# Gathering and scaling the next job's token rows at another place of a mixture-of-experts job loop

## What is computed

```python
x = attention(q, k, v, g_q, g_k)              # 4 batches, 12 heads, 448 tokens, 64 wide
x = x.transpose(0, 2, 1, 3).reshape(1792, 768)
# top-1 mixture of experts, 8 experts
expert = argmax(normalised(x) @ normalised(emb).T / tau); gate = softmax(...)[expert]
y = gate * (relu(x @ w1[expert]) @ w2[expert])   # w1: 768 x 1024, w2: 1024 x 768
# gated layer
out = (sigmoid(y @ w_gate) * (y @ w_val)) @ w_out
```

## Time and profile before

| | |
|---|---|
| median of 3 runs | 1223.03 us (1221.73 to 1224.38) |
| the profiled execution | 1228.75 us, its span 1227.2 us |
| TensorE (PE) busy | 1149.4 us, 94% of the span |
| VectorE (DVE), ScalarE (ACT), GpSimd (POOL) | 54%, 47%, 28% |
| attention to about 331 us, experts to about 669 us, layer 2 to the end | |

### The profile page before, as it was taken

One profiled execution on the slowest core, in us unless ns is written; L12 is line 12 of the kernel. 1 busy time (PEld: TensorE's weight loads), 2 busy tenths in 40 slices (PEclk: granted clock), 3 DMA queues, 4 the chain that ended last, 5 costly groups with the idle time before them and its releaser, 6 DMA issues. The chain is left out here.

```text
span 1227.2 us, 22232 instructions
## 1 busy us (share of the span) xinstructions
PE 1149.4 (94%) x7464; PEld 1005.1 (82%) x7465; DVE 658.5 (54%) x1136; ACT 576.8 (47%) x1282; POOL 347.9 (28%) x305
## 2 busy tenths in 40 slices
PE   4899999999669998999998999999999999999996
PEld 3566666666359998999998999999999999999995
DVE  4777777777755655565666343333333343333332
ACT  3777777777235544454555333233323333233321
POOL 7586767672362234323440000010001000010001
PEclk9999999999869999999999999999999999999998
DMA  3133432321157666766766434344333433343431
GB/s 80 36 103 99 123 95 72 89 62 46 23 134 198 185 175 164 193 186 179 205 181 161 132 103 111 105 140 117 112 103 111 139 103 103 103 147 105 117 105 51
DMA packets 255845, 147.12 MB, mean 120 GB/s; under 512 B 11128, under 2 KB 253048, under 8 KB 255808
## 3 DMA queue, kind: packets, MB, share of 16 engines
q1 hardware_dynamic: 251008, 132.25, 38.9%
q0 software_dynamic: 3872, 14.38, 4.1%
q10 hardware_dynamic: 928, 0.00, 0.0%
HBM read 135.52 MB, written 11.09 MB: 119 GB/s over the span
## 5 line engine op out<-in xcount | busy, mean ns | idle before, releaser
L1561 POOL DMA_INDIRECT out_dram<-rows,idp x16 | 18.0, 1125 | 561.6 <-DVE rows L1525 557.9
L1516 DVE TENSOR_TENSOR gv<-vb,sg 128x448 f32<-128x448 f32 x48 | 30.0, 625 | 219.8 <-PE vb L1579 203.8
L1349 PE MATMUL hb<-XH,W1H 128*128 128x256 f32 (+1 forms) x384 | 112.6, 293 | 16.4 <-issue 9.3
L727 ACT ACTIVATE PR<-sc,negmax 112x448 f32<-112x448 f32 x192 | 122.1, 660 | 0.0
L476 DVE TENSOR_REDUCE negmax<-sc 112x2 f32<-112x896 f32 x96 | 100.8, 1086 | 27.2 <-PE sc L836 26.9
L1349 PE MATMUL yb<-HH,W2H 128*128 128x256 f32 (+1 forms) x384 | 112.9, 294 | 0.0
L1472 ACT ACTIVATE l_WH<-stream 128x768 fp32r<-128x768 f32 x100 | 82.1, 839 | 62.3 <-PE vb L1579 60.9
L1577 PE MATMUL gb<-YH,l_WH 128*128 x288 | 107.1, 372 | 3.8 <-DVE l_WL L1509 3.6
L1351 PE MATMUL hb<-XH,W1L 128*128 128x256 f32 (+1 forms) x384 | 110.5, 288 | 0.0
L1350 PE MATMUL hb<-XL,W1H 128*128 128x256 f32 (+1 forms) x384 | 110.4, 288 | 0.0
L1350 PE MATMUL yb<-HL,W2H 128*128 128x256 f32 (+1 forms) x384 | 109.6, 285 | 0.0
(11 more groups left out here) (228 smaller groups left out, 2809.1 us busy)
## 6 DMA issues: line engine op xcount, KB each, us to landing
raw<-in_moe_w_dram SPq DMA_DIRECT2D x68, 384.0 KB, 4.8
stream<-in_moe_w_dram SPq DMA_DIRECT2D x48, 512.0 KB, 4.3
stream<-in_moe_w_gate_dram SPq DMA_DIRECT2D x34, 384.0 KB, 3.5
stream<-in_moe_w_val_dram SPq DMA_DIRECT2D x34, 384.0 KB, 4.1
stream<-in_moe_w_out_dram SPq DMA_DIRECT2D x32, 384.0 KB, 3.9
l_raw<-in_moe_w_gate_dram SPq DMA_DIRECT2D x16, 384.0 KB, 3.6
l_raw<-in_moe_w_val_dram SPq DMA_DIRECT2D x16, 384.0 KB, 4.2
l_raw<-in_moe_w_out_dram SPq DMA_DIRECT2D x16, 384.0 KB, 3.8
```

Source lines behind the costliest of these rows:

```text
L727: nc.scalar.activation(PR[:, h, j, :], sc[j % 2][0:P, h, 0:S], ACT.Exp, bias=negmax[:, s, j, h:h + 1], accum_out=den[:, s, h, j:j + 1]).th ...
L1349: nc.tensor.matmul(out[:, 0:n], WH[:, slot, k, :], mh, start=(k == 0), stop=False)
L1516: nc.vector.tensor_tensor(gv[:, f % 2, :], vb[f % 2][:, 0:S], sg[:, f % 2, :], ALU.mult).then_inc(prod, 1)
```

## The change

1. End of attention: VectorE builds the two matrices of the first of the four last tiles, then makes the gates, then builds the matrices of the other three.
2. SyncE waits, ahead of its first weight loads of job 0, until the rows of job 0 are turned.
3. The scaling of later jobs' rows goes from GpSimd to ScalarE (parts 0, 2) and VectorE (parts 1, 3), as a step `scale(j + 1)` between the last `h_out` and y 0. GpSimd keeps the index copy, the gathers and `store_ids`.
4. GpSimd waits, ahead of the index copy, until h 2 of job j is done too.
5. TensorE turns blocks 0 and 1 after y 0, block 2 after y 1, to block 5 after y 4; `x_out` moves likewise.

```diff
 finish():
-                for i in range(EARLY, TILES):
-                    chunk_of(i).then_inc(r.hi_l, 1)
-                    line_of(i).then_inc(r.lo_l, 1)
+                chunk_of(EARLY).then_inc(r.hi_l, 1)
+                line_of(EARLY).then_inc(r.lo_l, 1)
                 dve.wait_ge(r.exp_out, 1)
                 chain(nc.vector.tensor_reduce(r.gsum[:, :], r.EX[:, :, :], AX.X, ALU.add))
                 chain(nc.vector.tensor_scalar(r.gsum[:, :], r.gsum[:, :], 1e-9, None, ALU.add))
                 nc.vector.reciprocal(r.gate[:, :], r.gsum[:, :]).then_inc(r.gated, 1)
+                for i in range(EARLY + 1, TILES):
+                    chunk_of(i).then_inc(r.hi_l, 1)
+                    line_of(i).then_inc(r.lo_l, 1)
 SyncE:
-            rest_of(0, expert_of(sp, 1), 0)
+            following = expert_of(sp, 1)
+            sp.wait_ge(x_turned, KD)
+            rest_of(0, following, 0)
 job_order (ScalarE, VectorE):
-            x_out(j + 1, 0)
-            x_out(j + 1, 1)
+            scale(j + 1)
             for d in range(F2):
                 if d + 2 < F2:
                     w2_split(j, d + 2, 0)
                     w2_split(j, d + 2, 1)
                 y_out(j, d)
-                if d + 2 < F2:
-                    x_out(j + 1, d + 2)
+                if d == 0:
+                    x_out(j + 1, 0)
+                if d + 1 < F2:
+                    x_out(j + 1, d + 1)
                 if d in (3, 4):
                     w1_split(j + 1, d - 3)
 GpSimd:
                 pool.wait_ge(x_turned, KD * (j + 1))
                 pool.wait_ge(ids_out, 16 * (j + 1))
+                pool.wait_ge(h_done, SPLIT + F1 * j + 3)
...
                 fetch_rows(nc, c, x_rows)
                 store_ids(j + 1)
-                for a in range(4):
-                    pool.wait_ge(c.x_got[a], 16 * (j + 2))
-                    pool.sem_inc(x_arrived, 1)
-                    scale_rows(nc.gpsimd, a).then_inc(x_in, 1)
 ScalarE (VectorE alike, with a in (1, 3) and tensor_scalar):
+            def scale(j):
+                for a in (0, 2):
+                    act.wait_ge(c.x_got[a], 16 * (j + 1))
+                    nc.scalar.activation(xr[0:R, a, 0:DM], xr[0:R, a, 0:DM], ACT.Copy,
+                                         scale=xr[0:R, a, DM:ROW]).then_inc(gated_act, 1)
 TensorE:
                 if kd == 0:
-                    pe.wait_ge(x_in, 4 * j)
+                    pe.wait_ge(gated_act, 2 * (j + 1))
+                    pe.wait_ge(gated_dve, 2 * (j + 1))
...
-                turn(j + 1, 0)
-                turn(j + 1, 1)
                 for d in range(F2):
                     y(j, d, n)
-                    if d + 2 < KD:
-                        turn(j + 1, d + 2)
+                    if d == 0:
+                        turn(j + 1, 0)
+                    if d + 1 < KD:
+                        turn(j + 1, d + 1)
```

More of the change, by code:

```diff
@@ L1039, in experts @@
         yb = [ps(f"yb{i}", [128, 512]) for i in range(3)]
-        x_in = sem("x_in")
         raw1_in, raw2_in, w1_hi, w1_lo = c.raw1_in, c.raw2_in, c.w1_hi, c.w1_lo
@@ L1054, in experts @@
         x_asked = sem("x_asked")
-        x_arrived = sem("x_arrived")
         ids_out = sem("ids_out")
@@ L1132, in splits, with job_order @@
             return (count // ring) * j + (f // ring + 1)
-        def job_order(w1_split, w2_split, h_out, x_out, y_out, j):
+        def job_order(w1_split, w2_split, h_out, scale, x_out, y_out, j):
             for f in range(F1):
@@ L1155, in experts @@
         first_banks = tx + yb + hb[1:2]
-        def scale_rows(eng, a):
-            return eng.tensor_scalar(xr[0:R, a, 0:DM], xr[0:R, a, 0:DM], xr[0:R, a, DM:ROW], None, ALU.mult)
         @block.gpsimd
@@ L1218, in _ @@
             n_jobs = jobs(act, act.wait_ge)
-            for a in (0, 2):
-                act.wait_ge(c.x_got[a], 16)
-                nc.scalar.activation(xr[0:R, a, 0:DM], xr[0:R, a, 0:DM], ACT.Copy, scale=xr[0:R, a, DM:ROW]).then_inc(gated_act, 1)
+            def scale(j):
[3 more added lines that the diff above has]
+                                         scale=xr[0:R, a, DM:ROW]).then_inc(gated_act, 1)
+            scale(0)
             for kd in range(KD):
@@ L1229, in y_out @@
                     nc.scalar.activation(c.YH[:, d, bass.ds(s, T)], yb[d % YB][:, 0:T], ACT.Copy).then_inc(y_hi, 1)
-                job_order(w1_split, w2_split, h_out, x_out, y_out, j)
+                job_order(w1_split, w2_split, h_out, scale, x_out, y_out, j)
         @block.vector
@@ L1313, in _, with scale @@
             n_jobs = jobs(dve, dve.wait_ge)
-            for a in (1, 3):
-                dve.wait_ge(c.x_got[a], 16)
-                scale_rows(nc.vector, a).then_inc(gated_dve, 1)
+            def scale(j):
+                for a in (1, 3):
+                    dve.wait_ge(c.x_got[a], 16 * (j + 1))
+                    nc.vector.tensor_scalar(xr[0:R, a, 0:DM], xr[0:R, a, 0:DM], xr[0:R, a, DM:ROW], None,
+                                            ALU.mult).then_inc(gated_dve, 1)
+            scale(0)
             for kd in range(KD):
```

## The result

The change makes the kernel slower: 1237.49 us (median, 1236.73 to 1238.15) against 1222.38 beside it, ratio 1.0124, 95% interval 1.0104 to 1.0144. Forecast were 1213.7 and a range from 1208 to 1223.5.

What follows compares the result with a forecast made beforehand. TensorE was taken as the bound, so gains had to be its gaps. Terms -4.1 + 0.8 - 0.8 - 9.4 + 4.2 = -9.3 us took the median from 1223.03 to 1213.7, range 1208 to 1223.5.

Steps and rivals of the forecast that it cites:

- the rows in time: Ahead of turn 0 in six short jobs: rows arrive 0.7 us late each, +4.2 us, bounds 0 and 9.6.
- W1L waits: TensorE's waits for W1L at job ends and within jobs go: -9.4 us, other bound 0.
- Rival B: Job ends: YH is late for a reason that stays (loop, branch); -0.9 us, 1222.1, no change; chance 0.14.
- Rival A: Within jobs: late signal catches h 5, W1L waits ahead of h 7, 1.3 us per short job; 1217.3, faster; chance 0.22.
- C: Within jobs: hold catches h 4, waits ahead of h 6, 3.4 us per short job; 1234.9, slower; chance 0.13.
- D: Start of the experts: it doesn't move, block entry or VectorE's job table being next; 1216.7; chance 0.06.
- Start: Start of job 0: earlier gates and held weight loads bring TensorE's last turns forward, -4.1 us, bounds -3.3 and -4.8.
- Branches: First branch, beside released weight loads: +0.8 us (0 to +1.6); job 2's end, without the burst: -0.8 (0 to -1.6).
- The scaling moved off GpSimd: Between the last h_out and y 0: ScalarE's and VectorE's scaling fits under y 0's 2.83 us and costs nothing.

Runs made afterwards that it cites:

- The start alone: Kernel before with only the gates earlier and the weight loads of job 0 held until its rows are turned: 1217.72 us, ratio 0.9971; again 0.9966.
- before_d: Kernel before, unchanged, profiled once more on a third chip, one with prompt signals: 1221.49 us in that execution, 1221.0 in the median.

## Why the prediction was wrong

The failed step is **the rows in time**, +4.2 with an upper bound of 9.6; it measured +17.5 of waiting, and the clock, which was in no term, another 5 to 6. The demand was nearly right (turn 0 wanted 13.1 us after the split's start at 358.74, forecast 13.4). The supply was not: forecast were 13.5 us to the landing and 14.1 with the scaling, measured 15.7 to the turn. Three things add up. From release to the fourth issue it took 6.4 instead of 6.1; the issues of the four gathers take 1.38, 0.90, 1.15 and 1.15 us, where 0.91 was usual. The landing took 8.5 instead of 7.4, and 8.4 in the median of all. The rest, 0.2, is from the end of the scaling to the turn. I took the median of the earlier trace rows because both places have weight loads beside them; but those rows come from the job's end. With the same gathers one block earlier (the wait for h 1) the median landing is 6.7 us; why it is 8.4 behind h 2 is not shown. The shortfall was 0.7 us a job by the forecast, and every further us counts six times.

The Trainium skill, SBUF — State Buffer, section Who interferes with whom, holds that a VectorE instruction with both inputs in SBUF stands in the way of a GpSimd instruction that reads SBUF. The index copy agrees: 0.44 us at 359.45, inside a W1L split of VectorE that starts at 359.29 and takes 1.03, where the variant without the wait has 0.18. For descriptor writing beside such an instruction the page infers no conflict. The gathers beside VectorE's splits of W1 and W2, which both have two inputs in SBUF:

```profile
360.61 0.68 DVE L1299 TENSOR_TENSOR W2L<-stream,W2H 128x512 fp32r<-128x512 f32 x1
361.34 1.03 DVE L1239 TENSOR_TENSOR W1L<-raw,W1H 128x384 fp32r<-128x384 f32 x2
...
362.66 0.68 DVE L1299 TENSOR_TENSOR W2L<-stream,W2H 128x512 fp32r<-128x512 f32 x1
363.47 1.03 DVE L1239 TENSOR_TENSOR W1L<-raw,W1H 128x384 fp32r<-128x384 f32 x2
...
364.78 0.68 DVE L1299 TENSOR_TENSOR W2L<-stream,W2H 128x512 fp32r<-128x512 f32 x1
```

A split beside a gather does not lengthen it by itself: the fast one, 362.44 to 363.34, has the W2L split of 362.66 beside it. What the three slow ones share is a split that is already under way when they start (at 360.76, 363.64 and 365.10). All the traces here together bear that out: of 254 later-job gathers with a split under way 0.15 us after their start 230 took over 1.0 us, of 385 others 42. A gather also takes its index from SBUF (`xr<-x_rows,index`), so this does not contradict the page. And it is a coincidence in time only: no run here takes the splits away.

**The clock** was not in the sum at all. In the profile of before the only half-clock stretch behind the start of the experts lay at the branch of job 2's end, so I had no row for one behind a short wait.

**W1L waits, -9.4**: right as a reading of the trace and wrong for the measurement. The term is 9.4 on late chips, 1.0 on prompt ones. The sign was there: the profiled execution stood 5.7 above the median, and I carried that over as a constant offset, where it was mostly the very term that I meant to win. Rival B, late YH as a matter of the job's end, falls: moved with the burst, the hold left y 5 and met h 0. Rival A has its mechanism on late chips, and not its time: new waits for W1L lie ahead of h 7, 0.75 to 0.8 us in five of the six short jobs and 1.45 in the sixth (forecast 1.3), but the waits for rows shrink to 12.3 us and not to nothing, and the kernel is slower, not faster. C's waits ahead of h 6 came in no trace of the changed kernel. D falls with the start.

**Start, -4.1**: right. The start alone gives 3.5 and 4.1 us by its ratios (0.9971, 0.9966). In the changed kernel's trace:

```profile
344.83 0.62 DVE L1317 TENSOR_SCALAR xr<-xr 73x768 f32<-73x768 f32 x1 [1.03 <-DMA xr<-x_rows,index]
344.90 0.29 PEld L1393 LDWEIGHTS tx<-ident,xr 73*128 73x128 f32 x2 [0.27 <-ACT xr L1218]
...
346.66 0.99 SPq L1095 DMA_DIRECT2D raw<-in_moe_w_dram  x2
```

The last turns start at 344.90, forecast 344.1; attention's last step ahead of the gates (L686) lies at 329.30 here and at 327.96 in before's trace, so this execution was 1.3 us late already.

**Branches, +0.8 and -0.8**: they measured

```profile
L1399 PEldq COMPARE_BRANCH  x8: 87/218/3763, 346.4 to 636.3; - x8
```

```profile
L1401 PEldq COMPARE_BRANCH  x8: 73/76/4218, 350.2 to 636.6; - x8
```

against 3863 and 5495. Letting the held loads go beside the first branch cost nothing to be seen (3.76 us, and 3.91 in the changed kernel's second trace), so the upper bound was not reached. What the Trainium skill, Runtime: NRT & Kernel Launch, section Instruction fetch mechanics, states is only that a taken branch out of the fetched pages waits for a fetch; that other loads lengthen this fetch was the prediction's own step, and these rows don't show it. The second gained 1.3 in this pair of traces. TensorE's wait there is 4.8 to 5.3 us in the four traces of before and 3.9 to 4.2 in the three of the changed kernel, so 0.8 was about right.

The sum for prompt chips, from before_d's trace to the changed kernel's. Before_d's experts stage:

```profile
354.11:666.06 311.95, 302.87 (x2496) 301.74 (x2496) 192.51 (x386) 165.62 (x387) 112.70 (x77) 0.98 0.71 184
```

The first h product moves from 354.11 to 350.68, -3.4 (with the first branch in it). TensorE's idle time in the stage goes from 311.95 - 302.87 = 9.1 to 330.86 - 307.49 = 23.4, +14.3: 16.0 of waiting ahead of turn 0 by PE's own row, less 1.3 at the second branch and some small waits. Its busy time goes from 302.87 to 307.49, +4.6, and layer 2 from 553.9 to 553.7. The sum is +15.2, the difference of the spans (1235.2 - 1220.0), and the medians differ by 15.1. For late chips the stage of before and that of the changed kernel:

```profile
353.53:671.93 318.40, 302.67 (x2496) 299.92 (x2496) 196.36 (x386) 165.26 (x387) 112.61 (x78) 0.99 0.67 181
```

```profile
348.92:678.88 329.96, 307.04 (x2497) 303.44 (x2497) 196.57 (x402) 179.00 (x403) 43.73 (x48) 0.98 0.68 176
```

The first h product comes 4.6 us earlier, idle time grows by 7.2 (rows +12.3, W1L 9.4 to 6.1, 1.0 less at the second branch, the remainder small), busy time by 4.4, and layer 2 is 1.6 shorter: +5.4, the difference of the spans (1232.6 - 1227.2). The medians differ by 7.5 (1235.32 - 1227.87); these two profiled executions stand 1.3 below and 0.9 above theirs.

Two slips in the prediction's working changed nothing: C's threshold is (4.1 - 0.8 + 0.8 + 9.4) / 8 = 1.7 us a job, since 14.3 leaves out the first branch's +0.8; and a landing of 3.9 us gives -4.6 for the start and not -4.8, so that the lower bound, without a wait for rows, is 1209 and not 1208.

**The scaling moved off GpSimd** costs nothing, as forecast. It may be worth some 3 us: 0.9938 and 0.9944 without the wait, 0.9971 and 0.9966 for the start alone, the turns nothing by themselves. On late chips the two variants that differ only in who scales stand at 1.0047 and at 1.0075 and 1.0082. They ran on different chips, so this is not settled, and no row shows where the gain lies.

The version to keep waits for h 1: 0.9957 on a prompt and 0.9962 on a late chip. Without any wait it is 0.1 to 0.2% better on prompt chips (the intervals overlap) and 0.5% slower than before on a late one.

## What to carry to other kernels

If a change starts transfers on a trigger of its own, add up trigger, issue and landing with the worst rows of the stretch where they will lie, and leave a margin; here one product more of it, the wait for h 1, turned +1.2% into -0.4%. A short wait on TensorE costs more than its length when its clock falls behind it: here 15 us of waiting brought 6 us of slower matmuls. And when a profiled execution stands well above the median, find the rows that make the difference before you count them as a gain.

## What was not expected of the hardware

- Chips differ: on three of the five on which the experiments ran, a signal of TensorE that falls into the later part of GpSimd's DMA burst is acted on late (YH at 394.61 where TensorE had gone on to h 0 at 392.09), on two it never was in the traces; 6 to 8 us for the kernel before. The held signals were seen 1.1 to 1.2 us after the last gather's issue.
- The granted clock fell to 0.50 behind waits of 2.58, 3.27 and 3.13 us, but not behind one of 3.02, and, on a late chip, behind waits of 2.0 and 1.85 but not of 2.19: the length of a wait alone does not decide it.
- The same gather instruction is issued in 0.90 or in 1.15 to 1.38 us. In 230 of 254 cases a split of VectorE under way just after its start went with over 1.0 us.
